# Seven-product stage of an fp32 attention and MLP chain: first two x operands of a chunk made in steps of their own, the gated product's high part on ScalarE, the next stage's weights split around silu

## What is computed

```python
# attention: batch 4, heads 8, seq 576, head_dim 64
kv = einsum('bhsd,bhse->bhde', k, v)
out = einsum('bhsd,bhde->bhse', q, kv)
x = out / sqrt(mean(out * out, -1) + 1e-6) * g_norm      # -> 2304 x 512
# first MLP: d_model 512, d_ff 1536
g = x @ w_gate
x = ((g * (1 / (1 + exp(-g)))) * (x @ w_val)) @ w_out
# second MLP: d_ff 2048, softplus
h = x @ w_in2
return (maximum(h, 0) + log1p(exp(-abs(h)))) @ w_out2
```

## Time and profile before

| | |
|---|---|
| median of 3 runs | 926.0 us (925.85 to 926.09) |
| the profiled execution | 928.44 us, its span 926.4 us |
| mean granted TensorE clock | 0.982 of full |
| TensorE busy | 890.5 us, 96% of the span |
| VectorE, ScalarE, GpSimd busy | 686.2 (74%), 421.8 (46%), 229.6 us (25%) |
| chain that ended last | PE 90%, DVE 5%, ACT 1%, POOL 1%, issue 1%, DMA 1% |
| the stages in time | plain steps to 208 us, seven-product steps 208 to 520 us, second MLP from 522.5 us |

### The profile page before, as it was taken

How to read it: one execution, slowest core, us unless ns; L and a number is a source line. 1 busy time by engine, 2 the same in 40 slices (tenths; PEclk the granted TensorE clock), 3 DMA queues, 4 the chain that set the end, 5 groups by cost and what they waited for, 6 DMA issues and landing times.

```text
span 926.4 us, 14619 instructions
## 1 busy us (share of the span) xinstructions
PE 890.5 (96%) x5362; PEld 824.1 (89%) x5362; DVE 686.2 (74%) x1290; ACT 421.8 (46%) x742; POOL 229.6 (25%) x179
## 2 busy tenths in 40 slices
PE   8999999979899999979987899999999999999998
PEld 7999999979899999979976799999999999999997
DVE  3655656748967789887755799877877878878875
ACT  4617355744232333332222566554544544654553
POOL 4634104377801269921244200000000000000000
PEclk9999999989999999989999999999999999999999
DMA  9985865332100013110022220000000000000000
GB/s 269 214 224 136 162 129 143 92 114 69 46 1 1 1 35 92 36 34 1 1 69 92 69 69 24 34 0 0 34 0 0 34 0 0 34 0 0 35 1 35
DMA packets 95541, 53.93 MB, mean 58 GB/s; under 512 B 37248, under 2 KB 86528, under 8 KB 95488
## 3 DMA queue, kind: packets, MB, share of 16 engines
q1 hardware_dynamic: 95328, 53.23, 21.6%
q10 hardware_dynamic: 160, 0.00, 0.0%
HBM read 44.96 MB, written 8.26 MB: 57 GB/s over the span
## 4 chain that ended last, share of the span: by engine, by line
PE 90%; DVE 5%; ACT 1%; POOL 1%; issue 1%; DMA 1%; DVEq 0%; ACTq 0%; POOLq 0%; SPq 0%
PE bank L926 22%; PE bank L928 21%; PE bank L927 21%; PE bank L1085 7%; PE bank L1084 7%; PE bank L1083 7%; DVE gated L1577 1%; PE bank L866 1%; PE bank L859 1%; PE bank L934 1%; DVE g_lo L1590 1%; DVE ring L1541 1%; POOL slots L739 0%; ACT arena L1197 0%; PE bank L832 0%
## 5 line engine op out<-in xcount | busy, mean ns | idle before, releaser
L926 PE MATMUL bank<-x_hi,arena 128*128 128x384 f32 x554 | 188.1, 339 | 5.7 <-ACT act_a L1278 5.7
L928 PE MATMUL bank<-x_hi,arena 128*128 128x384 f32 x554 | 187.5, 338 | 0.0
L927 PE MATMUL bank<-x_lo,arena 128*128 128x384 f32 x554 | 186.9, 337 | 0.0
L926 PE MATMUL bank<-ring,slots 128*128 128x256 f32 x504 | 145.7, 289 | 19.1 <-DVE sum_b L1556 11.1
L928 PE MATMUL bank<-ring,slots 128*128 128x256 f32 x504 | 144.6, 287 | 0.0
L927 PE MATMUL bank<-ring,slots 128*128 128x256 f32 x504 | 144.4, 287 | 0.0
L1298 ACT ACTIVATE act_a<-bank 128x384 f32<-128x384 f32 x96 | 47.2, 492 | 179.2 <-PE bank L928 179.2
L926 PEld LDWEIGHTS bank<-ring,slots 128*128 128x128 f32 x504 | 98.2, 195 | 23.0 <-DVE sum_b L1556 12.3
L926 PEld LDWEIGHTS bank<-x_hi,arena 128*128 128x128 f32 x554 | 105.0, 190 | 10.0 <-issue 6.0
L1085 PE MATMUL bank<-arena,g_lo 128*128 128x512 f32 x288 | 113.1, 393 | 0.0
L1084 PE MATMUL bank<-arena,g_hi 128*128 128x512 f32 x288 | 112.9, 392 | 0.0
(11 more groups left out here) (139 smaller groups left out, 1675.0 us busy)
## 6 DMA issues: line engine op xcount, KB each, us to landing
stage<-in_moe_w_out SPq DMA_DIRECT2D x28, 256.0 KB, 3.6
out_dram<-out_stage SPq DMA_DIRECT2D x18, 256.0 KB, 2.1
k<-in_k SPq DMA_DIRECT2D x16, 256.0 KB, 3.2
v<-in_v SPq DMA_DIRECT2D x16, 256.0 KB, 3.5
stage<-in_moe_w_in SPq DMA_DIRECT2D x16, 256.0 KB, 2.8
xy<-in_q SPq DMA_DIRECT2D x48, 72.0 KB, 3.0
stage<-in_moe_w_gate SPq DMA_DIRECT2D x12, 256.0 KB, 3.7
stage<-in_moe_w_val SPq DMA_DIRECT2D x12, 256.0 KB, 3.9
```

The costliest lines, as they stand in the source:

```text
L926: nc.tensor.matmul(ps, hi, rhs_hi, start=first, stop=False)
L927: nc.tensor.matmul(ps, hi, rhs_lo, start=False, stop=False)
L928: return nc.tensor.matmul(ps, lo, rhs_hi, start=False, stop=last)
```

## The change

- `EARLY_OF` becomes `EARLY_AT`: operands 0 and 1 of a make are written one at a time, in steps k = 23 and 24 (make 1), q = 7 and 8 (make 2), 12 and 13 (make 3), 25 and 26 (make 4); before in q = 4, 9, 22, 27, both in one step.
- On GpSimd `x_sums` is cut in two. `first_x_sum` (two instructions, operand 1) of make 1 stands between the weights of f-blocks 1 and 2, and that of makes 2, 3, 4 right behind `x_sums` of the make before; a wait on a step's last product goes away.
- The high part of the gated product goes from VectorE (`split_g7`, L1588) to ScalarE (`g7_high`), behind `silu7_early` and the turn's operands and ahead of everything else of the step.
- `split_high2`: before two in one step between `keep_p1` and `silu7`; now the first there and the second behind `g7_high`.
- The low parts of the second MLP's weights on GpSimd are two instructions of 512 columns, before one of 1024.
- SyncE: the loads `load7_up(2)` and `load7_out(1)` stand ahead of `keep_x(3, 4)` and `fetch_x(3, 4)`, before behind them.
- TensorE: `up2(0, 0)`, the second MLP's first block, stands ahead of the last `down7`.

```diff
-EARLY_OF = {4: 1, 9: 2, 22: 3, 27: 4}
+EARLY_AT = {PLAIN - 1: (1, 0), PLAIN: (1, 1), PLAIN + 7: (2, 0), PLAIN + 8: (2, 1), PLAIN + 12: (3, 0), PLAIN + 13: (3, 1),
+            PLAIN + 25: (4, 0), PLAIN + 26: (4, 1)}
...
-HIGH2_AT = {5 * SEG + 1 + n // 2: ORDER2[n:n + 2] for n in range(0, SOON2, 2)}
+HIGH2_START = {5 * SEG + 1 + n // 2: ORDER2[n] for n in range(0, SOON2, 2)}
+HIGH2_END = {5 * SEG + 1 + n // 2: ORDER2[n] for n in range(1, SOON2, 2)}
...
@@ SyncE
-        for j in range(1, NT):
+        for j in range(1, NT - 1):
             keep_x(3, j)
             fetch_x(3, j)
-        for f in range(2, NF1):
+        load7_up(2)
+        load7_out(1)
+        keep_x(3, NT - 1)
+        fetch_x(3, NT - 1)
+        for f in range(3, NF1):
             load7_up(f)
             load7_out(f - 1)
...
@@ GpSimd
-        def x_sums(m):
-
-            t2, t3, t1, t4 = [in_blocks(x7_sum(m, i)) for i in (1, 2, 3, 5)]
+        def first_x_sum(m):
+
+            t2 = in_blocks(x7_sum(m, 1))
             pool.wait_ge(x_ready, X_NEEDED7[CHUNK_OF_MAKE[m]])
-            if m:
-                pool.wait_ge(p_done, product_count(LAST_STEP_OF_MAKE[m - 1] - 3, SEVEN - 1))
             wait_x7_place(m, 1)
             nc.gpsimd.tensor_tensor(t2, x_block(m, 1, 1), x_block(m, 0, 1), ALU.subtract).then_inc(x_sum_ready, 1)
             pool.wait_ge(x_sum_ready, 6 * m + 1)
             nc.gpsimd.tensor_tensor(t2, t2, x_block(m, 0, 0), ALU.add).then_inc(x_sum_ready, 1)
+
+        def x_sums(m):
+
+            t3, t1, t4 = [in_blocks(x7_sum(m, i)) for i in (2, 3, 5)]
...
+        first_x_sum(0)
         x_sums(0)
         for f in range(SEG):
             weight_sums(f)
             weight_lows(f)
+            if f == 1:
+                first_x_sum(1)
         x_sums(1)
+        first_x_sum(2)
         x_sums(2)
+        first_x_sum(3)
         for f in range(SEG, NF1):
             weight_sums(f)
             weight_lows(f)
         x_sums(3)
+        first_x_sum(4)
         x_sums(4)
         for f in ORDER2[:SOON2]:
             wait_slot2(pool, f)
-            low(high_count2(f), arena[:, slots2[f]:slots2[f] + SLOT2], stage2[:, ORDER2.index(f) % 2, :], RAW2)
+            pool.wait_ge(w_hi_ready, high_count2(f))
+            for o in range(0, RAW2, KT * P):
+                at = slots2[f] + o
+                last = nc.gpsimd.tensor_tensor(arena[:, at + RAW2:at + RAW2 + KT * P],
+                                               stage2[:, ORDER2.index(f) % 2, o:o + KT * P],
+                                               arena[:, at:at + KT * P].bitcast(F32), ALU.subtract)
+            last.then_inc(w_ready, 1)
...
@@ TensorE
+        pe.wait_ge(value_early_ready, STEPS7)
+        up2(0, 0)
         down7(STEPS7 - 1)
-        for f in range(LAG2):
+        for f in range(1, LAG2):
             up2(0, f)
...
@@ ScalarE
+        def g7_high(q):
+
+            act.wait_ge(g_ready, PLAIN + q + 1)
+            act.wait_ge(g_late_ready, q + 1)
+            if q >= 2:
+                act.wait_ge(down_done, PLAIN + q - 1)
+            nc.scalar.activation(g7_hi[:, q % 2, :], gated[:, :], ACT.Copy).then_inc(g_hi_ready, 1)
...
             keep_p1(q)
-            for f in HIGH2_AT.get(q, ()):
-                split_high2(f)
+            if q in HIGH2_START:
+                split_high2(HIGH2_START[q])
             silu7(q)
...
-            if q in EARLY_OF:
-                for i in range(2):
-                    x7_high(EARLY_OF[q], i)
+            g7_high(q)
+            if k in EARLY_AT:
+                x7_high(*EARLY_AT[k])
+            if q in HIGH2_END:
+                split_high2(HIGH2_END[q])
             if q == 0:
                 store_y(NC1 - 1)
...
@@ VectorE, split_g7
-            nc.vector.tensor_copy(g7_hi[:, q % 2, :], gated[:, :]).then_inc(g_hi_ready, 1)
             dve.wait_ge(g_hi_ready, PLAIN + q + 1)
...
@@ VectorE, the steps
             split_g7(q)
-            if q in EARLY_OF:
-                for i in range(2):
-                    x7_low(EARLY_OF[q], i)
+            if PLAIN + q in EARLY_AT:
+                x7_low(*EARLY_AT[PLAIN + q])
```

More of the change, by code:

```diff
@@ L1646, in _ @@
                 x7_low(0, FIRST_X7_AT[k])
+            if k in EARLY_AT:
+                x7_low(*EARLY_AT[k])
         for q in range(STEPS7):
```

## The result

The changed kernel takes 899.17 us (median of 4 runs, 897.63 to 900.18); the kernel before took 926.05 beside it (925.85 to 928.98). The ratio is 0.9701, 95% interval 0.9677 to 0.9725. The profiled execution took 897.63 us, with a span of 895.9 us against 926.4.

A forecast was written before the change was run, and what follows sets the result against it. TensorE, busy for 96% of 926.4 us, bounds the kernel, so only its waits and slow clock give time back. Gains of 39.5 less 13.2 of new waits make 26.3: 926.0 becomes 899.7 us, range 889 to 912.

The forecast's parts named there:

- A: Plain step 23: TensorE's wait for a silu behind a late weight load, and the slow clock after, go; gain 8.0 us.
- B: Seven-product step 5: excess time from two VectorE operands in one step, colliding with GpSimd, goes; gain 5.6 us.
- C: Seven-product step 23: excess time from two VectorE operands in one step, colliding with GpSimd, goes; gain 7.3 us.
- D: From step 32 to the second MLP: excess time, with weight blocks ahead of silu, goes whole; gain 18.6 us.
- E: Steps 0 and 1: ScalarE's queue and GpSimd's added sums make TensorE wait 3.6 us, plus 2.0 of slow clock.
- F: Turns, steps 6, 12, 24 and 30: two more GpSimd sums delay VectorE's burst of operands; loss 6.8 us in all.
- G: Steps 18 and 22: second-half weights come late as ScalarE's part starts later; 0.4 us of wait each, 0.8 in sum.
- The first: Rival: VectorE slips between the sums at the turns, or TensorE doesn't feel it; 893 us; chance 0.25.
- The second: Rival: the queue behind the moved copy costs its upper bounds, 25 us; gain 14.4, 911.6 us; chance 0.12.
- The copy on the path in each step: Rival: the copy on ScalarE adds 0.20 us in 36 steps, 7 us; gain 19, 907 us; chance 0.03.
- the slower case: Rival: keep_p1 queues late behind the copy in every seven-product step, 1.2 us a step; 930 us; chance 0.02.
- nothing moves: Rival: the waits only change their names, which needs new waits of 39.5 us; chance 0.02.

The follow-up runs named there:

- u_sync: The changed kernel with SyncE's two weight loads back behind keep_x(3, 4) and fetch_x(3, 4): 906.41 us, 0.9813 of the kernel before.
- u_early: The changed kernel with operands 0 and 1 of a make in one step again and GpSimd's first sums in their old places: 900.05 us, ratio 0.9725.
- d_only: The kernel before, with only the second block of second-MLP weights moved behind the silus: 907.3 us, ratio 0.981.
- u_silu: The changed kernel with both second-MLP weight blocks of a step ahead of the silus again: 920.83 us, ratio 0.9965.
- u_half: The changed kernel with GpSimd's low part of a second-MLP weight block in one instruction again: 900.22 us, ratio 0.9723.
- u_cast: The changed kernel with the copy of the gated product's high part back on VectorE: 900.46 us, ratio 0.9732.
- x_sum_late: The changed kernel with GpSimd's first sums of makes 2, 3 and 4 held until the last product of the step behind the turn: 894.35 us, ratio 0.967.
- keep_first: The changed kernel with GpSimd's first sums held back and ScalarE's keep_p1 ahead of store_y(1), accumulator emptying and the weight highs of steps 0 and 1: 889.54 us, 0.9613.

## Why the prediction was right, and where it was not

**A, 8.0 us: right.** The load is issued at 184.64 (I said near 186), ScalarE waits 0.50 us for it and runs the part at 188.96. T0 gained 7.0 us by `u_sync` and 7.8 by the two profiles, without the 1.3 us that arise earlier.

**B and C, 5.6 and 7.3: right to the tenth,** and `u_early` brings 4.5 and 5.6 of it back; what is missing can be the copy, which stays off VectorE there. `u_early` puts operands and sums back together, so the share of GpSimd's collisions was not tried by itself. That both sizes fit to the tenth needed only that the two steps fall to 7.78 us.

**D, 18.6: right, and its cause shown** by `d_only` and `u_silu`. By the two profiles it is 17.7, and with the 0.9 of steps 34 and 35 that I had not foreseen 18.6. The spare of half a us was real: in step 35 the first block ends at 486.01, and the silu of that half starts at 486.51:

```profile
484.95 1.06 ACT L1221 ACTIVATE arena<-stage 128x1024 fp32r<-128x1024 f32 x1 [1.31 <-DMA stage<-in_moe_w_out]
486.51 0.42 ACT L1268 ACTIVATE gated<-gated 128x256 f32<-128x256 f32 x1 [0.51 <-DVE gated L1601]
```

"Halving L696 halves what one collision can cost" holds for one instruction (`u_half`); I did not see that the second half catches the next instruction of the same chain, so that nothing is saved where both are on it (`u_silu`).

**"The copy itself costs nothing in a usual step": right.** No step without a turn, an early weight or a weight block is longer than 7.79 us. The chain did grow by more than the 0.20 us of the two copies. Before, the last product ended at 474.47 and the low part began at 474.97; in the changed kernel VectorE stands still for 0.80 us between them:

```profile
482.55 0.69 DVE L1625 TENSOR_TENSOR g_lo<-gated,g_hi 128x512 fp32r<-128x512 f32 x1 [0.80 <-ACT g_hi L1257]
```

That is 0.30 us more: 0.20 for the copy (0.63 for 0.43) and 0.10 for the way to ScalarE and back. The prediction counted no such way; the cover of 4 us hid it.

**E, 3.6 of wait and 2.0 of slow clock: too large.** The waits are 0.85 and 1.75, the steps 3.1 us longer. In step 0 the cause is as given (in `u_early`, without `first_x_sum(1)` in that place, the wait is gone): the weight sums wait behind `first_x_sum(1)` on GpSimd, and ScalarE waits for them:

```profile
193.67 1.61 POOL L764 TENSOR_TENSOR ring_sums<-xy 128x512 f32<-128x512 f32 x1
195.36 1.36 POOL L766 TENSOR_TENSOR ring_sums<-ring_sums,xy 128x512 f32<-128x512 f32 x1
...
200.18 1.06 ACT L1233 ACTIVATE slots<-slots_sums 128x1024 fp32r<-128x1024 f32 x1 [4.01 <-POOL slots_sums L735]
```

I had taken 1.6 between 0.2 and 3.0. In step 1 the size was right (2.0 for 1.75), but the queue behind the copy is not the only cause (`u_cast`). The slow clock is missing in this profile and costs 1.5 us in half of the profiles with the same wait, so a flat 2.0 was too much. Its rate of 0.57 us for each us of wait was not all clock either: at 0.24 us for each of the ten waits of the earlier trace rows, about 2.4 of those 10.7 us (an estimate from step 6) come at any clock.

**F, 6.8: mechanism right, size 5.6.** The turn of step 5, GpSimd's first sum (the 1.48 and 1.36) and VectorE beside it:

```profile
246.60 1.48 POOL L764 TENSOR_TENSOR ring_sums<-xy 128x512 f32<-128x512 f32 x1
248.16 1.36 POOL L766 TENSOR_TENSOR ring_sums<-ring_sums,xy 128x512 f32<-128x512 f32 x1
...
246.85 1.51 DVE L1616 TENSOR_TENSOR gated<-gated,sum_a 128x256 f32<-128x256 f32 x1
248.28 2.45 DVE L1581 SCALAR_TENSOR_TENSOR ring<-ring_sums,gain,ring 128x512 fp32r<-128x512 f32 x2
```

In `x_sum_late`, with GpSimd idle there, the same two groups take 0.41 and 1.40 us:

```profile
246.65 0.41 DVE L1618 TENSOR_TENSOR gated<-gated,sum_a 128x256 f32<-128x256 f32 x1
246.98 1.40 DVE L1583 SCALAR_TENSOR_TENSOR ring<-ring_sums,gain,ring 128x512 fp32r<-128x512 f32 x2
```

So the two sums cost VectorE 1.10 + 1.05 = 2.15 us, where I gave them their whole length, 2.6. Each VectorE instruction that suffers begins 0.1 to 0.25 us after GpSimd's, and stands for about what is left of it. The turn is late by 2.0 and not by 2.4. The Trainium skill (SBUF — State Buffer, "Who interferes with whom") says that a VectorE instruction with two SBUF inputs contends with a GpSimd instruction that reads SBUF, and calls the shared port pair an exclusive lock. The rows agree: with 1.48 - 0.25 = 1.23 us of GpSimd's instruction left, L1616 takes 1.10 us longer. The prediction took the whole length of GpSimd's instruction; VectorE's late start is what it left out.

**G, 0.8: right** (0.83 in steps 18 and 22), with 0.34 more in steps 17 and 21 that I had not listed. All four go in `u_cast`, so they need the copy on ScalarE.

**The sum.** Forecast 39.5 - 13.2 = 26.3. By the two profiles the gains are 7.8 + 5.6 + 7.3 + 18.6 = 39.3 and the new pieces 9.9 + 0.9 = 10.8; 1.3 + 0.6 us come from stages that the change leaves alone, so the spans differ by 30.5. The medians differ by 26.9, because the profiled execution of before stood 2.4 us above its median and that of the changed kernel 1.5 below. The forecast of 899.7 lies 0.5 from the median. A part of that closeness is chance: the step that was off is the size of the new waits (13.2 for 10.8). With the terms as measured, 39.3 - 10.8 = 28.5, the same sum would have said 897.5, and how the two profiled executions stand to their medians fills the gap. Some of those 1.5 us is probably the slow clock of step 1, absent in the profile and, by their mean clocks, present in the other executions; then the 2.0 us of E were less wrong for the median than for this profile.

**Rivals.** The first (TensorE doesn't feel the turns) is refuted by the nine waits in steps 6, 12 and 24. The second's queue exists, but costs 9.9 of its 25 us up to step 30. The copy on the path in each step, the slower case and "nothing moves" did not come.

What stays open: whether step 35's small wait is more than where GpSimd's block happens to fall, and what decides if the clock falls behind a wait as in step 1.

## What to carry to other kernels

On an engine whose queue feeds the bound engine, put the instruction that frees the bound engine first and let optional work (weight preparation, emptying accumulators, output stores) queue behind it: one such move gave 17 of the 27 us here (`d_only`), and a few more, with a GpSimd sum held back, another 9.6 (`keep_first`). Count a moved GpSimd instruction at its new place too, since it slows whatever VectorE runs beside it: making the x operands in separate steps saved 10 us in two steps and gave 7 back in step 0 and at three turns. And compare a profiled execution with the median of its kernel before adding up spans: here the spans differ by 30.5 us and the medians by 26.9.

## What the runs showed of the hardware that was not expected

- The same wait of 1.75 us in the same place of the same kernel was followed by a granted clock of 1.00 in one execution and 0.67 (down to 0.50) in another; it costs 1.5 us or nothing. In step 5 it was so too: 1.00 behind 2.60 us in `d_only`, 0.50 behind 2.58 us before, for 2.8 us of difference.
- A wait of TensorE between matmuls of 256 columns costs about 0.24 us more than its bracket, at a full clock: 2.02 us for three waits of 1.31 us, 2.00 for one of 1.75, 1.08 for one of 0.85.
- GpSimd's work in two instructions costs a chain on VectorE 2.80 us in two successive instructions, and whole 2.44 + 0.41 = 2.85: the same. Where one instruction of the chain is exposed, it takes 1.69 us beside the halves in place of 2.79 beside the whole, and 0.56 undisturbed.
